# Layer 1's last four chunks by seven products, attention as one pipeline in five chunks, and w_in sums made in portions

## The reference, cut to what matters

```python
# q, k, v: [8 batches, 8 heads, 576, 64]
k_p = k.reshape(B, H, 72, 8, D).mean(axis=3)          # keys and values pooled by 8
v_p = v.reshape(B, H, 72, 8, D).mean(axis=3)
attn = softmax(q @ k_p.T / sqrt(D))
x = (attn @ v_p) -> [4608 tokens, 512]

h = np.maximum(x @ w_in, 0.0)                          # layer 1: 512 -> 2048
x = h * h @ w_out                                      #          2048 -> 512

h = x @ w_in2                                          # layer 2
g = where(h >= 1, h, where(h <= -1, 0, (h + 1)**2 / 4))
out = g @ w_out2
```

## Time and profile before

| | us |
|---|---|
| time, median of 3 runs (1715.77 to 1718.85) | 1716.84 |
| the profiled execution's own time | 1716.59 |
| its span, first to last instruction | 1714.8 |
| one layer-1 chunk with a batch of attention beside it | 107.7 |
| one layer-1 chunk without attention (the last two) | 88.8 and 88.7 |
| one pair of layer 2, a and b | 108.8 + 54.4 |

### The profile page before, as it was taken

The page is one execution under the profiler, slowest core; times in us unless marked ns, Lnnn a source line. Parts: engine busy times, 40 slices in busy tenths (PEclk is TensorE's granted clock), DMA queues, the critical chain, the costliest instruction groups (busy, mean ns, idle before and its releaser), DMA issues.

```text
span 1714.8 us, 23006 instructions
## 1 busy us (share of the span) xinstructions
PE 1701.4 (99%) x8182; PEld 1374.1 (80%) x8182; DVE 871.0 (51%) x1415; ACT 688.8 (40%) x1213; POOL 229.2 (13%) x255
## 2 busy tenths in 40 slices
PE   9999999999999999999999999999999999999999
PEld 7777777777777777777888788888888888888887
DVE  6664434434344343443544556556465746566552
ACT  5443333333333333333334434444354435444441
POOL 5333313223132231320000000000000000000000
PEclk9999999999999999999999999999999999999999
DMA  6544232232232332324653502332333232233310
GB/s 172 140 137 126 85 96 78 65 100 87 85 88 66 100 87 73 99 66 162 236 213 128 190 1 82 144 110 108 111 128 129 84 140 103 115 116 111 129 68 25
DMA packets 119645, 187.92 MB, mean 110 GB/s; under 512 B 40704, under 2 KB 77056, under 8 KB 114432
## 3 DMA queue, kind: packets, MB, share of 16 engines
q1 hardware_dynamic: 119552, 186.68, 33.5%
HBM read 135.27 MB, written 51.38 MB: 109 GB/s over the span
## 4 chain that ended last, share of the span: by engine, by line
PE 95%; DVE 2%; issue 1%; ACT 1%; DMA 1%; SPq 0%; POOL 0%; DVEq 0%; ACTq 0%; POOLq 0%
PE ps_y L1292 44%; PE ps_h L1250 25%; PE ps_a L1317 9%; PE ps_h L1317 8%; PE ps_a L1200 2%; PE ps_a L1224 2%; PE ps_a L1237 2%; PE ps_a L1214 1%; DMA wq_raw<-in_moe_w_in 1%; PE ps_y L1132 0%; DVE sq_f L932 0%; PE ps_a L1149 0%; DVE probs L872 0%; PE ps_y L1170 0%; ACT act_f L701 0%
## 5 line engine op out<-in xcount | busy, mean ns | idle before, releaser
L1250 PE MATMUL ps_h<-xc,w_hi 128*128 128x512 f32 x1264 | 399.2, 397 | 0.0
L1292 PE MATMUL ps_y<-w_hi,g_hl 128*128 128x512 f32 x1152 | 388.9, 389 | 1.5 <-ACT stage L721 1.5
L1292 PE MATMUL ps_y<-g_hl,w_hi 128*128 128x512 f32 x1152 | 365.6, 398 | 1.9 <-DVE g_hl L936 1.9
L932 DVE TENSOR_TENSOR sq_f<-act_f 128x512 f32<-128x512 f32 x144 | 108.5, 753 | 392.1 <-ACT act_f L701 392.1
L1250 PEld LDWEIGHTS ps_h<-xc,w_hi 128*128 128x128 f32 x1264 | 230.7, 188 | 52.9 <-issue 9.2
L1292 PEld LDWEIGHTS ps_y<-g_hl,w_hi 128*128 128x128 f32 x1152 | 209.6, 188 | 57.3 <-issue 16.5
L1292 PEld LDWEIGHTS ps_y<-w_hi,g_hl 128*128 128x128 f32 x1152 | 216.2, 188 | 46.9 <-DVE w_lo L861 1.9
L1250 PE MATMUL ps_h<-xc,w_lo 128*128 128x512 f32 x632 | 247.3, 391 | 0.0
L1292 PE MATMUL ps_y<-g_hl,w_lo 128*128 128x512 f32 x576 | 225.3, 391 | 0.0
L1292 PE MATMUL ps_y<-w_lo,g_hl 128*128 128x512 f32 x576 | 224.1, 389 | 0.0
L701 ACT ACTIVATE act_f<-ps_h 128x512 f32<-128x512 f32 x144 | 86.0, 597 | 335.4 <-PE ps_h L1250 334.5
(11 more groups left out here) (146 smaller groups left out, 1874.8 us busy)
## 6 DMA issues: line engine op xcount, KB each, us to landing
xc<-w_in_ops SPq DMA_DIRECT2D x32, 1792.0 KB, 7.2
xc<-attn_out_hl SPq DMA_DIRECT2D x32, 512.0 KB, 4.2
attn_out_hl<-xo_hl SPq DMA_DIRECT2D x56, 288.0 KB, 2.2
out<-stage SPq DMA_DIRECT2D x36, 256.0 KB, 3.2
stage<-in_moe_w_in SPq DMA_DIRECT2D x32, 256.0 KB, 3.7
stage<-in_moe_w_out SPq DMA_DIRECT2D x32, 256.0 KB, 4.7
mlp_out_hl<-stage SPq DMA_DIRECT2D x32, 256.0 KB, 2.4
w_in_ops<-wq_hl SPq DMA_DIRECT2D x8, 1024.0 KB, 5.7
```

The lines of the kernel that those rows point to most:

```text
L932: nc.vector.tensor_tensor(sq_f[:, f % 2, :], act_f[:, f % 2, :], act_f[:, f % 2, :], ALU.mult).then_inc(square_done, 1)
L1250: mm = nc.tensor.matmul(ps_h[:, f % 2, :], left[:, f, kd * P:(kd + 1) * P], xc[:, buf, right, kd, :], start=(kd == 0 and n == 0), stop=(kd ...
L1292: mm = nc.tensor.matmul(ps_y[:, m, :], left, right, start=(f == 0 and n == 0), stop=(f == NF - 1 and n == 2))
```

## The change

Three things, and what follows from them.

1. Layer 1's chunks 5 to 8 are two pairs with seven products (`PLAIN = 5`, `NPAIR1 = 2`), by the code of layer 2's pairs with layer 1's activation (no `bend`, `take_y` on ScalarE where layer 2 has `take_out` on VectorE). Attention's output of those chunks is stored once as fp32 (`attn_out`, from `xo_raw`) instead of as high and low parts. Chunk 4 also prepares the first pair's 14 operand tiles (`pair_ops`, `op_high`), as chunk 9 does in layer 2.
2. Attention of batches 1 to 7 is one pipeline of 56 units in 171 slots. They are put at groups, a group being three matmuls of a step's 24: slot s comes after group `s * 600 // 171` counted from chunk 0, so every three or four groups, and the last one lies in chunk 4's step 10. On VectorE and ScalarE all slots of a step now stand ahead of `hidden1(f + 2)`.
3. The operands of w_in and w_in2 are made in 32 portions (`prep_high`, `prep_low`, half the rows of one column pair each), in two of every three steps from chunk 1 step 2 to chunk 4 step 0, after the step's slots and ahead of `hidden1`. There is one raw buffer and one result buffer: portion n + 1's load waits until portion n is done, and ScalarE's first copy of n + 1 waits until both stores of n have landed.

Layer 2's weights are now split in chunk 8 at one per step of 12 matmuls (`split_w(NF + f - 2)`), from eight staging places that overlay the chunk buffer xc; places 8 to 15 are loaded after `load_y` and `load_raw`.

```diff
-    SLOTS = 3 * NU + 3
+    PLAIN = 5
+    NPAIR1 = (NC - PLAIN) // 2
+    UNITS = NU * (B - 1)
+    SLOTS = 3 * UNITS + 3
+    GROUPS = 2 * MT
+    SPREAD = {5: 600, 3: 364}[PLAIN]
+    UNIT_PLACES = [(NF + 2 + 3 * n // 2) for n in range(2 * NF)]
...
+        def slots_at(c, f, group):
+            at = (c * NF + f) * GROUPS + group
+            return [s for s in range(SLOTS) if s * SPREAD * 10 // (10 * SLOTS) == at]
+        def step_slots(c, f):
+            return [s for group in range(GROUPS) for s in slots_at(c, f, group)]
...  SP, chunk 8 (b of the last pair of layer 1)
+                elif layer == 1:
+                    for n in range(8):
+                        load_second(n)
+                (store_y if layer == 1 else store_out)(a)
...
+                elif layer == 1:
+                    sp.wait_ge(w_ready, NF + 4 - 2)
+                    for hp in range(KD):
+                        load_y(NC, 1, hp)
+                    sp.wait_ge(g_ready, (NC - 1) * NF + 2 * KD)
+                    load_raw(2, True, At(NC + 1))
+                    for n in range(8, NF):
+                        load_second(n)
...
             def load_wq(n):
+                layer, fp, j = n // NF, n // 2 % NP, n % 2
+                if n:
+                    sp.wait_ge(wq_ready, 4 * n)
+                sp.dma_start(raw_w.rearrange("p (h c) -> p h c", h=2), (w_in, w_in2)[layer]...[fp, j]
+                             ).then_inc(wq_loaded, DMA)
...  ScalarE
+            def prep_high(n):
+                act.wait_ge(wq_loaded, DMA * (n + 1))
+                if n:
+                    act.wait_ge(wq_stored[0], DMA * n)
+                    act.wait_ge(wq_stored[1], DMA * n)
+                raw = raw_w.rearrange("p (h c) -> p h c", h=2)
+                nc.scalar.copy(first_hl[:, 0, 0:2, :].bitcast(F32R), raw[:, :, 0:P]).then_inc(wq_hi_done, 1)
+                nc.scalar.copy(wa_hl[:, 0, 0, :], raw[:, 1, P:2 * P]).then_inc(wq_hi_done, 1)
+                act.wait_ge(wq_sum_done, 4 * n + 4)
+                nc.scalar.copy(first_hl[:, 0, 2:4, :].bitcast(F32R), sum_w[:, 0:2, :]).then_inc(wq_hi_done, 1)
+                nc.scalar.copy(wa_hl[:, 0, 1:3, :], sum_w[:, 2:4, :]).then_inc(wq_hi_done, 1)
...  VectorE: prep_low(n) has four sums of 128x128, then low parts of 256, 128, 256 and 256 columns
...  ScalarE and VectorE, chunk
+                    if fixed == PLAIN - 1 or fixed == NC:
+                        pair_ops(layer, True, At(0 if layer == 1 else NPAIR1), f - 2)
+                    if layer == 1:
+                        for s in step_slots(fixed, f):
+                            attention_slot(s)
+                        n = prep_unit(fixed, f)
+                        if n is not None:
+                            prep_low(n)
+                    if f + 2 < NF:
+                        (hidden2 if layer == 2 else hidden1)(c, f + 2)
...  in pair, b's loop over f
+                    elif layer == 1 and f >= 2:
+                        split_w(NF + f - 2)
...  TensorE
+                for f in range(NF - 2 if last else NF):
+                    for group in range(GROUPS):
+                        if group < MT:
+                            output(c, f, layer, [group])
...
+                            hidden(c, buf, f + 2, ..., [group - MT])
+                        if layer == 1:
+                            for s in slots_at(fixed, f, group):
+                                attention_slot(s)
...
-            chunk(At(0), 0, True, 1)
-            with pe.Fori(0, (NC - 3) // 2) as i:
-                chunk(At(1, i, 2), 1, True, 1)
-                chunk(At(2, i, 2), 0, True, 1)
-            chunk(At(NC - 2), 1, False, 1)
-            chunk(At(NC - 1), 0, False, 1)
+            for c in range(PLAIN):
+                chunk(At(c), c % 2, 1)
+            pair_step(1, At(PLAIN - 1), NF - 2, At(0), At(0), 0)
+            for p in range(NPAIR1):
+                pair(1, At(p), At(PLAIN + 2 * p), p + 1 < NPAIR1)
```

More of the change, by code:

```diff
@@ L206, in pv_unit @@
             if s == SLOTS - 1:
[L207 to L214, removed]
-        def kv_count(b, which, hp):
-            return b.times(2 * KD, KV_ORDER.index((which, hp)) + 1 - 2 * KD)
+                return UNITS - 1
+            return w - 2 if r == 0 and w >= 2 else None
@@ new lines, in kv_slots, with plain_cols, store_parts @@
+        def kv_slots(table, s):
+            return [(b, n) for b in range(1, B) for n in range(2 * KD) if s == max(3 * NU * (b - 1) + table[n], 0)
+                    and not (table is KV_LOAD_SLOT and b == 1 and n < 2)]
+        def kv_count(b, which, hp):
+            return 2 * KD * (b - 1) + KV_ORDER.index((which, hp)) + 1
+        def plain_cols(w):
+            b, u = unit(w)
+            return min(max(PLAIN * CHUNK - b * S - (u % 2) * HALF, 0), HALF)
+        def store_parts(w):
+            return (plain_cols(w) > 0) + (plain_cols(w) < HALF)
@@ new lines, in x_count, with x_needed @@
+        def x_count(w, par):
+            return DMA * ((KD if par else 0) + sum(store_parts(v) for v in range(w + 1) if v % 2 == par))
+        def x_needed(last, hp, par):
+            b = (last - par * HALF) // S
+            return DMA * KD * par if b < 1 else x_count(NU * (b - 1) + 2 * hp + par, par)
+        def slots_at(c, f, group):
[3 more added lines that the diff above has]
+            return [s for group in range(GROUPS) for s in slots_at(c, f, group)]
@@ L474, in _ @@
+                (store_y if layer == 1 else store_out)(a.plus(1))
             first_load_k(0)
@@ L806, in chunk @@
                         take_y(c)
[L807 to L816 removed]
+                    if layer == 1:
+                        for s in step_slots(fixed, f):
+                            attention_slot(s)
+                        n = prep_unit(fixed, f)
+                        if n is not None:
+                            prep_high(n)
@@ L879, in attention_slot @@
-                if r == 2 and u < NU:
-                    dve.wait_ge(exp_done, b.times(NU, u + 1))
-                    nc.vector.tensor_reduce(stat[:, u % 2, 1, :], groups(probs[:, u % 2, :]), AX_X,
+                if w is not None and plain_cols(w):
+                    n = plain_cols(w)
+                    dve.wait_ge(x_hi_done, NU + sum(plain_cols(v) > 0 for v in range(w + 1)))
+                    nc.vector.tensor_tensor(xo_hl[:, w % 2, 1, 0:n], bank_b[:, 0:n],
+                                            xo_hl[:, w % 2, 0, 0:n].bitcast(F32), ALU.subtract).then_inc(x_split, 1)
@@ L982, in diff @@
+            def diff(layer, first, p, o, j):
                 dve.wait_ge(raw_loaded, p.times(2 * DMA, 2 * DMA))
@@ L1084, in chunk @@
-                    if c.at(NC):
-                        pair_ops(True, At(0), f - 2)
-                    if attention:
-                        for s in chunk_slots(f, 0):
-                            attention_slot(c.plus(1), s)
-                    if not (layer == 2 and f + 2 >= NF):
-                        ahead = c if f + 2 < NF else c.plus(1)
-                        second = layer == 2 or (c.at(NC - 1) and f + 2 >= NF)
-                        (hidden2 if second else hidden1)(ahead, (f + 2) % NF)
@@ L1097, in _ @@
+                    if f + 2 < NF:
+                        (hidden2 if layer == 2 else hidden1)(c, f + 2)
+                    elif layer == 1 and fixed + 1 < PLAIN:
+                        hidden1(c.plus(1), f + 2 - NF)
             for u in range(NU):
@@ L1342, in chunk @@
[L1342 to L1356 removed]
+                        pair_step(layer, a, 2 * s)
```

841 lines of the change are left out of this document (449 added, 392 removed).

## The result

The changed kernel takes 1722.74 us (median of 8 runs, 1720.79 to 1728.14) where the kernel before takes 1717.07 (8 runs): ratio 1.0035, 95% interval [1.0026, 1.0044]. It is slower by 0.35%; I had forecast 1710, faster.

What follows compares the result with a forecast made beforehand. TensorE's stream was taken as the bound. 1685.1 us without new stalls, plus 10.5 (P slots), 2.4 (chunk 0), 5.0 (chunk 4) and 5.5 (layer 2's weights) gave 1708.5 span, 1710.3 with 1.8 beyond it; forecast 1710, range 1693 to 1725.

Steps and rivals of the forecast that it cites:

- Matmuls taken out: Layer-1 pairs: 336 product matmuls each where there were 384, saving 21.8 us in all; each pair takes 163.2 us.
- rival D: Layer-1 pairs stall because `take_y` and weight splits sit on ScalarE: 2 to 4 us per pair, 1716; chance 0.07.
- P slots behind sums of weights: P slots wait for scores where a portion follows a Q slot: ten places, 10.5 us.
- The step that failed: Portions behind a P or S slot: the next user's need comes a slot later, so no stall, 0 us.
- The portion's VectorE time: A portion's eight VectorE operations, with two waits on ScalarE's copies, take 2.15 us.
- the lock: VectorE operations with two SBUF inputs and GpSimd's SBUF reads exclude each other: 4 us more, left out of the sum.
- Chunk 0: In steps 3 and 7, `hidden1` and a weight split on VectorE delay scores: stalls of 2.4 us, bounds 0 and 5.
- Chunk 4: In steps 6 to 10, differences or low parts ahead of slots stall P and S slots: 5.0 us, bounds 0 and 10.
- Layer 2's weights: Chunk 8: place 8's load comes late in the queue; ScalarE waits 7 to 8 us, TensorE stalls 5.5.
- a base of 1685.1: Span without new stalls: 1714.8 less 21.8 for matmuls, 6.7 for old stalls and 1.2 for merged attention.
- B: Rival: portions run late as a chain and all 32 cost; at 1.0 us each 1732, slower; chance 0.12.
- One free step in three: Argument against crowding by portions: they occupy two of every three steps, leaving one free; no size given.

Runs made afterwards that it cites:

- e2_no_portions: Changed kernel without the 32 portions of weight sums (no loads, copies, sums or stores; operands come from other data): 1700.31 us.
- the experiment: Changed kernel with GpSimd's first two adds for every k and v cut to 8 columns: 1712.0 us.
- the small stores: Changed kernel with each of a portion's two stores cut to 64 KB, its loads, copies and sums kept: 1715.88 us.
- the halves: Changed kernel with each portion cut in two, sums and low parts around different slots, same work and traffic: 1711.45 us.

## Why the prediction was wrong, by its own steps

- **Matmuls taken out**: right. The first pair takes 108.80 + 54.40 = 163.2, the three hand-overs stall nothing, and **rival D** did not come.
- **P slots behind sums of weights**: for what it counted, right. Forecast 10.5 us in ten places; measured 11.7 in eight, 0.6 to 1.0 in the single ones and 1.6 to 3.5 where stores were waited for. That the total is so near is in part luck: two places stalled nothing and one stalled 3.5.
- **The step that failed** is the sentence "After a P or an S slot the next user's need comes a slot later and I find no stall". With a portion behind a P slot, the S slot that comes two slots later waited in five places, 3.6 us, for the Q slot's output to be taken; with a portion behind an S slot, the Q slot two later waited for the P slot's copy in seven, 6.7 us. I had looked only for the S-to-P distance; but every slot overwrites a bank whose content, written by the slot just before it, VectorE or ScalarE must have taken, and the portion stands ahead of that taking whichever kind of slot it follows. 10.3 us at nothing. One more S slot, at the end of chunk 3, stalled 1.4 us; it does so without portions too (`e2_no_portions`).
- **The portion's VectorE time** was mis-sized: 2.15 us, measured 3.8 on average from its first operation to its last, 3.0 without most of GpSimd's adds. I had the lock at 4 us beside the sum, from one pair of rows; the experiment gives up to 10.7, for portions, `hidden1` and chunk 0 together.
- **Chunk 0**: 2.4, measured 4.3: the P slots of steps 3 and 7 took 2.6 of it, as forecast, and a P slot in step 12 and two short waits the rest. **Chunk 4**: 5.0, measured 2.7, two P and S slots in steps 6 and 7.
- **Layer 2's weights**: right. ScalarE waits once, 6.3 us for 7 to 8; TensorE 4.7 for 5.5.
- **The clock** was missing: 0 for 6.9 in the profiled execution. A stall was priced at its length; behind it came half to three quarters as much again where the clock fell. It is also one reason why the executions spread over 7 us where those of before spread over 3: the slowest has the lowest mean clock, 0.994, the others 0.996 to 0.999.
- In sum: 23.4 us forecast, 30.4 + 4.7 + 6.9 = 42.0 in the profiled execution, on a base of 1685.1 that held within 1 us. The median lies 5.4 lower, which leaves some 13 us of error. 10.3 of it are the failed step. The rest is what the other errors come to: the 1.4 of the S slot in chunk 3, 1.9 too little for chunk 0 and 1.2 for the P slots, 2.3 too much for chunk 4 and 0.8 for layer 2, and some 1.5 that the clock left in the median, if the 5.4 are the clock's. Of the rivals B came true: the portions cost 22.4 / 32 = 0.70 us each, its break was 0.53, and it had a chance of 0.12. B's "for it" (single buffers, two waits per portion) was a part of the mechanism, 6.9 us by the small stores; the length of the block, which the halves show, was more. "One free step in three" helped too little: ScalarE still waited for stores twelve times.

## What to carry to other kernels

When work is packed beside a pipeline of slots, list for every slot the buffer it needs and who must leave it, and put the block of added work behind each kind in turn; the kind you know from the old trace is one of several. Here a block of 3.8 us cost 22 us in 32 places; cut in two, it left half of the slot stalls. Spread over five chunks for three it left almost none, which was worth more than the 10.9 us of matmuls given up as long as the blocks were whole, and no more once they were cut in two. Price a stall of TensorE of some 2 us or more above its length (here by half to three quarters, where the clock fell), and put the load that is wanted first ahead in its queue.

## What the runs showed of the hardware

In the changed kernel's profile the granted clock fell to 0.50 at stalls of 1.9 to 4.7 us and cost 1.4 to 2.4 us each time. At the one for g_hl it fell in all six profiles that had it open; at stalls of slots of 1.9 to 3.6 us it fell in some profiles and not in others; with matmuls on zeros in the stall for g_hl it did not fall, in one profile. The Trainium skill ("TensorE: Matmul & The Clock Gate", Part 1) describes the lower clock as the default that activity lifts; the rows agree in its level. VectorE's 128-column sum took 0.28 us, and 1.38 beside GpSimd's add.
